# Attention and two feed-forward layers on one core: a second set of probability buffers in the first unit, new instruction orders, short heads' q in two halves

## The reference

```python
scores = scale * np.matmul(q, k.transpose(0, 1, 3, 2)) + bias      # 4 sequences, 8 heads, 576 rows, head_dim 64
scores = scores - np.max(scores, axis=-1, keepdims=True)
attn = np.exp(scores)
attn = attn / (np.sum(attn, axis=-1, keepdims=True) + 1e-09)
x = np.matmul(attn, v)                                             # as 2304 tokens x 512
h = x @ w_in                                                       # layer 1, 512 -> 2048 -> 512
y = (h - np.tanh(h)) @ w_out
g = y @ w_gate                                                     # layer 2, 512 -> 1536 -> 512
out = (g * (1.0 / (1.0 + np.exp(-g))) * (y @ w_val)) @ w_out2
```

## Time and profile before

| | us |
|---|---|
| median of three runs | 1268.38 (1267.01 to 1269.97) |
| the profiled execution's own time | 1264.43 |
| its span, first to last instruction | 1262.6 |
| TensorE busy | 1185.2 (94%) |
| VectorE busy | 635.8 (50%) |
| ScalarE busy | 576.3 (46%) |
| GpSimd busy | 540.2 (43%) |
| mean granted clock of TensorE | 0.991 |

### The profile page before, as it was taken

The page is one execution under the profiler, slowest core; times in us unless marked ns, Lnnn a source line. Parts: engine busy times, 40 slices in busy tenths (PEclk is TensorE's granted clock), DMA queues, the critical chain, the costliest instruction groups (busy, mean ns, idle before and its releaser), DMA issues.

```text
span 1262.6 us, 20294 instructions
## 1 busy us (share of the span) xinstructions
PE 1185.2 (94%) x7312; PEld 1094.9 (87%) x7312; DVE 635.8 (50%) x1401; ACT 576.3 (46%) x1171; POOL 540.2 (43%) x600
## 2 busy tenths in 40 slices
PE   5767699999999999999999999999999999999998
PEld 2346688999999998999899999999999999999998
DVE  8966776666556556777777734521211212112111
ACT  6965566655555555555555544521212222122212
POOL 2046566755555555777777733211111111111111
PEclk9998899999999999999999999999999999999999
DMA  5886455343444433444444334300000001000000
GB/s 176 265 247 181 128 171 178 107 141 104 119 122 129 118 108 117 132 128 128 146 136 127 102 135 147 125 26 1 26 26 25 25 13 39 1 26 1 26 1 26
DMA packets 80068, 125.47 MB, mean 99 GB/s; under 512 B 19424, under 2 KB 42976, under 8 KB 79968
## 3 DMA queue, kind: packets, MB, share of 16 engines
q1 hardware_dynamic: 79968, 124.17, 32.5%
HBM read 104.07 MB, written 20.05 MB: 98 GB/s over the span
## 4 chain that ended last, share of the span: by engine, by line
PE 64%; DVE 18%; issue 8%; ACT 8%; SPq 1%; DMA 1%; DVEq 0%; POOL 0%; ACTq 0%
PE ps_s L1341 12%; PE ps_y L1352 12%; PE ps_y L1271 9%; PE ps_h L1252 8%; PE ps_h L1341 6%; PE ps_pt L1341 6%; DVE prob L993 5%; PE ps_pt L1208 4%; DVE fr L967 3%; DVE feat L960 3%; PE ps_pt L1225 2%; ACT wbuf L738 2%; DVE wbuf L1009 2%; PE ps_s L1192 2%; DVE g_b L1020 2%
## 5 line engine op out<-in xcount | busy, mean ns | idle before, releaser
L669 POOL TENSOR_TENSOR fr<-tanh_b,fr 128x384 fp32r<-128x384 f32 x72 | 73.0, 1014 | 378.1 <-ACT fr L890 378.1
L1271 PE MATMUL ps_y<-fr,wbuf 128*128 128x384 f32 x1152 | 226.2, 337 | 2.0 <-ACT xy_stage L777 1.3
L617 POOL TENSOR_SCALAR prob<-prob,rowinv 128x576 f32<-128x576 f32 (+1 forms) x160 | 127.8, 799 | 207.6 <-DVE rowinv L1004 190.9
L1252 PE MATMUL ps_h<-fr,wbuf 128*128 128x384 f32 x1056 | 206.8, 340 | 1.8 <-DVE g_b L1020 1.8
L1271 PEld LDWEIGHTS ps_y<-fr,wbuf 128*128 128x128 f32 x1152 | 198.8, 188 | 2.6 <-POOL fr L622 2.6
L1252 PEld LDWEIGHTS ps_h<-fr,wbuf 128*128 128x128 f32 x1056 | 182.1, 189 | 3.1 <-DVE g_b L1020 2.8
L731 ACT ACTIVATE prob<-prob,negmax 128x576 f32<-128x576 f32 (+1 forms) x160 | 124.1, 776 | 103.8 <-DVE negmax L993 102.6
L1352 PE MATMUL ps_y<-wbuf,fr 128*128 128x512 f32 x648 | 161.1, 393 | 0.0
L622 POOL TENSOR_TENSOR fr<-g_b,fr 128x384 fp32r<-128x384 f32 x96 | 108.4, 1129 | 110.9 <-ACT fr L755 110.9
L1352 PEld LDWEIGHTS ps_y<-wbuf,fr 128*128 128x128 f32 x648 | 120.5, 188 | 22.1
L1009 DVE TENSOR_TENSOR wbuf<-ps_pt,wbuf 128x512 fp32r<-128x512 f32 (+1 forms) x144 | 97.0, 674 | 58.6 <-ACT wbuf L738 57.5
(11 more groups left out here) (128 smaller groups left out, 1994.9 us busy)
## 6 DMA issues: line engine op xcount, KB each, us to landing
biasb<-bias_scratch SPq DMA_DIRECT2D x128, 216.0 KB, 2.6
raw<-k_t SPq DMA_DIRECT2D x59, 288.0 KB, 2.8
bias_scratch<-w_raw SPq DMA_DIRECT2D x72, 144.0 KB, 3.3
biasb<-bias_scratch SPq DMA_DIRECT2D x64, 144.0 KB, 2.9
w_raw<-w_chunks SPq DMA_DIRECT2D x16, 512.0 KB, 5.4
prob<-w_chunks SPq DMA_DIRECT2D x8, 768.0 KB, 4.2
raw<-v_p SPq DMA_DIRECT2D x32, 160.0 KB, 2.3
biasb<-bias_scratch SPq DMA_DIRECT2D x64, 72.0 KB, 2.6
```

What stands on the lines that cost most here:

```text
L617: eng.tensor_scalar(row, row, rowinv[0:hd.rows, tile % PR:tile % PR + 1], 1.0, ALU.mult, ALU.mult).then_inc(p_norm, 1)
L1252: mm = eng.matmul(hidden_bank(u, c)[:, 0:TOK], w[:, cols], x[:, d, :], start=d == 0 and i == 0, stop=d == KC - 1 and i == 2)
L1271: mm = eng.matmul(ps_y[:, d, 0:TOK], w[:, cols], g[c % 2], start=c == 0 and i == 0, stop=c == C1 - 1 and i == 2)
```

## The change

The probability buffers exist twice in unit 0: even heads below 8 use a second set in a part of `wbuf` that W1 fills later, and `pt_high` waits for the output two heads back. All engines get new orders in the slots of attention alone (`alone`), and the ninth slot (`edge`) finishes head 7 ahead of most of head 8. In the slots of layer 1 with long heads, `q_low` goes ahead of the last `score`, and the W1 splits move: two ahead of the first exponential, two to the slot's end. In a unit's first slot `y_out` is issued in parts. In short slots q of consecutive heads goes to alternating halves of `qq`, so `q_high` and `q_low` come early in the slot, and q is loaded ahead of the bias. In the last unit TensorE runs two hidden chunks ahead of the model chunks rather than one. Near the end of the bias stage, the loads of bias tiles 4 and 5 go ahead of the last two stores of bias.

Buffers and helpers:

```diff
         tail = C1 * 2 * W1C
         k_hi = wbuf[:, tail:tail + S]
...
-        pt_end = wbuf[:, pt_at:pt_at + TOK]
+        pt_bufs = []
+        for pt_at in (tail + S, (C1 - 2) * 2 * W1C):
+            pt_bufs.append([wbuf[:, pt_at + i * FULL * TOK:pt_at + (i + 1) * FULL * TOK] for i in range(2)]
+                           + [wbuf[:, pt_at + 2 * FULL * TOK:pt_at + 2 * FULL * TOK + TOK]])
...
+        def pt_second(hd):
+            return hd.n < H and hd.n % 2 == 0
+        def pt_free(hd):
+            return hd.n - 1 if hd.n < H else hd.n
...
         def operands(hd, moe):
...
+            if not ended(hd):
+                at = hd.n % 2 * width(hd)
+                return qq[:, at:at + width(hd)], k_hi, k_lo
...
+        def preparing_q(hd, moe):
+            if ended(hd) or ended(HEADS[hd.n - 1]):
+                return preparing(hd, moe)
+            return HEADS[hd.n - 1].tile0
```

SyncE's queue:

```diff
             for rnd in range(1, NQUAD, 2):
+                if rnd >= NQUAD - 4:
+                    load_bias(BR + (rnd - (NQUAD - 4)) // 2)
                 store_bias(rnd)
...
-            for n in range(H):
+            load_bias(BR + 2)
+            for n in range(1, H):
...
             for n in range(H, NH):
                 hd = HEADS[n]
                 load_v(hd)
+                following = HEADS[n + 2:n + 3]
+                for nxt in following:
+                    if not ended(hd):
+                        load_q(nxt)
                 for t in range(hd.nt):
+                    if t == 0 and hd.unit > 1 and n == FIRST_OF[hd.unit] + 1:
+                        store_y(hd.unit - 2, 0)
                     load_bias(hd.tile0 + t + BR)
...
+                    if t == 1 and hd.unit > 1 and n == FIRST_OF[hd.unit] + 1:
+                        store_y(hd.unit - 2, 1)
```

GpSimd, the slots of attention alone:

```diff
                 if not moe:
+                    edge = q.n == H
+                    if edge:
+                        split_v(v)
                     if p is not None:
                         split_k(p, moe)
-                    if v is not None:
-                        split_v(v)
                     for t in range(q.nt):
                         norm(q, t)
+                        if t == 0 and v is not None and not edge:
+                            split_v(v)
```

ScalarE:

```diff
+            def alone(q, v, p, moe):
+                for t in range(q.nt):
+                    if v is not None:
+                        pt_high(v, t, moe)
+                    if t == 0 and p is not None:
+                        q_high(p, moe)
+                    exp_tile(q, t)
+                if v is not None:
+                    pt_high_end(v)
+                if q.n >= 2:
+                    o_part(HEADS[q.n - 2], moe)
...
+            def edge(q, v, p, moe):
+                for t in range(v.nt):
+                    pt_high(v, t, moe)
+                o_part(HEADS[v.n - 1], moe)
+                pt_high_end(v)
+                eng.wait_ge(e_score, q.tile0 + 1)
+                x_high(0)
+                exp_tile(q, 0)
+                o_part(v, moe)
+                q_high(p, moe)
+                exp_tile(q, 1)
...
+            def dense_alone(moe):
+                u, s = moe[0][0], moe[0][1] // 2
+                for (u, c), splits in zip(moe, w2_plan(s)):
+                    if c == 0:
+                        y_out(u - 1)
+                    tanh(u, c)
+                    g_high(u, c)
+                    for k in splits:
+                        w2_high(k)
...
+            def short(q, v, p, moe):
...
+                pt_high(v, 0, moe)
+                if first:
+                    y_out(u - 1, [0])
+                if p is not None:
+                    q_high(p, moe)
+                if q is not None:
+                    exp_tile(q, 0)
+                if not first:
+                    tanh(u, c)
+                pt_high(v, 1, moe)
...
+                u, tiles, first = moe[0][0], w1_tiles(moe), begins(moe)
+                pt_high(v, 0, moe)
+                if v.n == H:
+                    exp_tile(v, 2)
+                for k in tiles[-1:] + tiles[0:1]:
+                    w1_high(k)
+                if first:
+                    y_out(u - 1, [0])
+                exp_tile(q, 0)
...
+                o_part(v, moe)
+                if late(moe):
+                    x_high(u + 1)
+                for k in tiles[1:3]:
+                    w1_high(k)
```

VectorE:

```diff
+            def alone(q, v, p, moe):
+                for t in range(q.nt):
+                    score(q, t, moe)
+                    if t == 1 and p is not None:
+                        q_low(p, moe)
+                    if v is not None:
+                        pt_low(v, t, moe)
+                    if t > 0:
+                        inverse(q, t - 1)
+                if v is not None:
+                    pt_low_end(v)
+                if q.n >= 2:
+                    x_out(HEADS[q.n - 2], moe)
+                inverse(q, q.nt - 1)
...
+            def short(q, v, p, moe):
...
+                pt_low(v, 0, moe)
+                if q is not None:
+                    score(q, 0, moe)
+                if p is not None:
+                    q_low(p, moe)
+                if q is not None:
+                    inverse(q, 0)
+                if not first:
+                    gated(u, c)
+                pt_low(v, 1, moe)
+                if q is not None:
+                    score(q, 1, moe)
...
+                x_out(v, moe)
+                if q is not None:
+                    inverse(q, 1)
...
+                pt_low(v, 0, moe)
...
+                score(q, 0, moe)
+                for k in tiles[0:1]:
+                    w1_low(k)
...
+                pt_low(v, 2, moe)
+                if not first:
+                    q_low(p, moe)
+                for t in range(2, q.nt):
+                    score(q, t, moe)
...
+                pt_low_end(v)
...
+                gated(*moe[1])
+                x_out(v, moe)
+                for k in tiles[1:3]:
+                    w1_low(k)
```

TensorE:

```diff
+            def alone(q, v, moe):
+                for t in range(q.nt):
+                    if t == 2 and q.n >= 2:
+                        output(HEADS[q.n - 2], moe)
+                    scores(q, t, moe)
...
+                    if v is not None:
+                        transposed(v, t, moe)
+                if v is not None:
+                    transposed_end(v, moe)
...
+            def edge(q, v, moe):
+                for t in range(v.nt):
+                    transposed(v, t, moe)
+                output(HEADS[v.n - 1], moe)
+                transposed_end(v, moe)
+                scores(q, 0, moe)
+                scores(q, 1, moe)
+                output(v, moe)
+                scores(q, 2, moe)
...
+            def dense_alone(u, c):
+                if c == 0:
+                    pieces = model_pieces(u - 1, C1 - 1) + hidden_pieces(u, 0) + hidden_pieces(u, 1)
+                else:
+                    pieces = (hidden_pieces(u, c) + model_pieces(u, c - 2)
+                              + hidden_pieces(u, c + 1) + model_pieces(u, c - 1))
+                for piece in pieces:
+                    piece()
...
+                gaps = [4, 4, 2] if len(moe) == 2 else [4, 2]
+                if moe[0] == (0, 0):
+                    layer_work(4)
+                    gaps = [0, 0, 2]
```

More of the change, by code:

```diff
@@ new lines, in slot @@
+                g_high(*moe[0])
+                exp_tile(q, 1)
+                if first:
+                    y_out(u - 1, [3])
+                else:
+                    pt_high(v, 2, moe)
+                q_high(p, moe)
+                pt_high_end(v)
+                for t in range(2, q.nt):
+                    exp_tile(q, t)
+                tanh(*moe[1])
+                g_high(*moe[1])
+                o_part(v, moe)
+                if late(moe):
+                    x_high(u + 1)
+                for k in tiles[1:3]:
+                    w1_high(k)
@@ L1108, in slot @@
-                if not one:
-                    x_out(v, moe)
-                for k in tiles[2:3]:
+                    dense_alone(moe)
+                    return
+                if len(moe) == 1:
+                    short(q, v, p, moe)
+                    return
+                u, tiles, first = moe[0][0], w1_tiles(moe), begins(moe)
+                pt_low(v, 0, moe)
+                if v.n == H:
+                    inverse(v, 1)
+                    inverse(v, 2)
+                score(q, 0, moe)
@@ L1123, in _ @@
             eng.sem_inc(v_t, 1)
-            slots(slot, edge)
+            slots(slot)
             def y_low(v, par):
```

357 lines of the change are left out of this document (156 added, 201 removed).

## The result

| | before | after |
|---|---|---|
| median of the runs, us | 1267.70 (1263.24 to 1269.97) | 1247.30 (1247.15 to 1248.48) |
| profiled execution, us (its span) | 1264.43 (1262.6) | 1247.15 (1245.3) |
| mean granted clock | 0.991 | 0.992 |

The ratio is 0.9845, with a 95% interval of 0.9817 to 0.9873: 1.5% faster. The prediction was 1243.4 us, in a range of 1233 to 1256. In the profiled pair the gain is 17.3 us of span, where the sum said 25.0; the medians fell by 20.4.

What follows compares the result with a forecast made beforehand. TensorE was taken as the bound from about 158 us on, with waits left elsewhere, chiefly in attention alone. Gains summed to 25.0 us: 1264.4 - 25.0 = 1239.4 profiled, 1243.4 as a median, range 1233 to 1256.

Steps and rivals of the forecast that it cites:

- Short slots: Short slots of layer 1: early `q_low` stops delaying `x_out`; 28 slots x 0.33 = 9.2 us gained, bounds 0 and 10.
- last unit: Last unit: another hidden chunk covers waits of 1.26 and 0.73 us; 2.3 us gained, bounds 1.5 to 2.6.
- Start: Start of attention alone: earlier load of tile 4's bias saves half of a 4.01 us wait; 2.1 us gained.
- Attention alone: Heads 3 to 7: second buffer set cuts the ring, period 9.09 falls to 8.2 us; 4.5 us gained.
- Ninth slot and edge: Ninth slot and unit 0's first slot: head 7 finished first, some 25 us instead of 28; 2.9 us gained.
- the exposed three: `q_low`, `w1_low` and `x_low`: the only operations listed as open to delay by the port pair VectorE shares with GpSimd.
- Unit 0: Unit 0's six other slots with W1 work: moved W1 splits gain 0.46 of 0.96 us each, 2.8 us.
- the first score chain is as late as before: Unit 0's slots: `w1_low` ahead of the first `inverse` waits for GpSimd's W1 split, limiting the gain to 2.8 us.
- Long slots of units 1 and 2: 14 slots without the two first ones: `q_low` ahead of the third score loses nothing if VectorE gets the ports first; 0.
- rival (a): Long slots: GpSimd gets the ports first every time, output 0.5 us later, 14 slots 7 us, 1250; chance 0.21.
- rival (b): GpSimd keeps the ports over both halves of k, delaying outputs in long slots and unit 0: 40 us, 1283; chance 0.07.
- First slots: First slots of units 1 to 4: `y_out` in parts ends a 0.66 us wait; 1.2 us gained, short units 0.

Runs made afterwards that it cites:

- the run with the stores late: Changed kernel with the last two bias stores (eight issues) moved behind SyncE's loads for head 2; 1248.83 us, ratio 0.986.
- The run with a later `q_low`: Changed kernel with `q_low` in attention alone moved behind the third score's `pt_low` and `inverse`; 1243.86 us, ratio 0.9813.
- the run with `q_low` late: Changed kernel with `q_low` back behind `pt_low_end` in all long slots of layer 1; 1244.47 us, ratio 0.9821.
- the filler: TensorE computes each head's first score four times over in attention alone: on the changed kernel 1246.76 us, on that kernel with three repairs 1250.92 us.

## Why the prediction was right, and where it was not

**Short slots** (9.2, measured 9.0) and **last unit** (2.3, measured 2.6): the mechanism was right in both. The short slots were read off a row of before in which the cost was absent, the last slot without a q; the sum counted 28 of them where there are 27. The two waits of the earlier trace rows in the last unit are gone.

**Start** (2.1, measured 2.6): the size is right, and tile 4 is scored at 77.07, as said. The reason given for the half that stays, the pace of the loads, is half right. At tile 6 VectorE's own chain stands right behind the loads; at tile 7 a bias is still 1.11 us late, which falls into the next term (the run with the stores late). The score of tile 6 came at 83.43 to 85.45 in kernels that start alike, so the 0.5 us over the forecast can't be told from chance.

**Attention alone** (4.5, measured 2.2): the mis-sized term. The period is 8.67, not 8.2. The waiting for the ports was right (0.66 to 0.79 against 0.8); `pt_high_end` is 0.58 instead of 0.3, the clock 0.2 to 0.4 instead of 0.1. With VectorE's 7.0 these make 8.6. The run with a later `q_low` shows that the kernel could have spared 0.72 a slot.

**Ninth slot and edge** (2.9, measured 1.1): the order is worth 2.1 by itself, and 1.0 is lost among the other edits. Part of that is in the first slot of layer 1, where TensorE has four waits of 0.99 to 1.62 us (4.7 in all). The first and the last of them, and what stands before the first on VectorE and GpSimd, in the changed kernel:

```profile
145.57 2.73 PE L1378 MATMUL ps_h<-fr,wbuf 128*128 128x384 f32 x12 [0.99 <-DVE fr L1115]
...
154.43 1.09 PE L1334 MATMUL ps_pt<-ident,prob 128*128 128x128 f32 x4 [1.62 <-DVE wbuf L1086]
...
142.86 2.57 DVE L1115 TENSOR_TENSOR fr<-xy_stage,fr 128x1152 fp32r<-128x1152 f32 x1
...
142.78 1.43 POOL L627 TENSOR_TENSOR fr<-raw,wbuf 128x576 fp32r<-128x576 f32 x1
```

`x_low` begins 0.08 us after GpSimd's low half of k and takes 2.57 us; in the run with the old edge the same instruction takes 1.36. The prediction named `x_low` among the exposed three and put no price on it. TensorE waits 0.99 us for it, so that is the most it can cost. That it does is argued from the rows: no run took it away with the new order kept, and in the run with the later `q_low` the edge takes 30.73 us with an `x_low` just as long, so other waits move it as much. How the gain divides between this term and the one before hangs on the cut: set at head 6's output they are 2.1 and 1.1 us, the other way round. Together they are 3.3 of the 7.4 forecast.

**Unit 0** (2.8, measured 4.8): the step that failed is "the first score chain is as late as before". From a slot's first score to its second `pt_low` the changed kernel takes 2.55 us (192.11 to 194.66) and 2.56 (205.95 to 208.51) in the two kinds of slot, where before it took 3.29 (185.08 to 188.37). The early split does wait for GpSimd in every second slot, but VectorE would have waited for the exponential there, so the first `inverse` is only 0.14 us later. What the prediction said of the splits at the end is half right: in every second slot they and GpSimd's `norm` press on each other, and 0.5 of the 1.0 us is lost again. By the run with `q_low` late, 0.25 of a slot's gain is that of the early `q_low`.

**Long slots of units 1 and 2** (0, measured -3.1): the step that failed is the choice between forecast and rival (a). The prediction's own sign of being wrong, an output in unit 1 that waits for `pt_low_end`, is there in 12 of these 14 slots (0.23 to 0.29 us). GpSimd was first in all 14, by about 0.1 us. The price was 0.35 a slot in ten of them and 0.1 in the last two, where the rival had 0.5; the run with `q_low` late has it back. The second slot of each unit gained 0.35 (14.0 to 13.65). The argument "a waiting VectorE got its turn at once" was right, but it concerns the turn between two instructions of GpSimd, not who is first. It is why rival (b) did not come: GpSimd's low half at 322.83 took 1.60 us behind the waiting `q_low`, where it takes 1.43 with nobody ahead of it.

**First slots** (+1.2, measured -1.3): `y_out` in parts did cut its wait, from 0.66 to 0.20 us, but the change also puts `split_g` behind GpSimd's second `norm` in these slots, and 0.93 us of waiting for it is new. I read that edit and gave it no cost. This step was an omission, not a wrong size. The first two slots of unit 3, taken at 0, lost 0.6: the first output there waits 0.74 us for a `pt_low` where it waited 0.22. No run took that apart.

The Trainium skill (SBUF — State Buffer, SBUF: two separate sides) says that an operation which takes the pair holds it for its whole length. Here the traces agree: `q_low` 0.56 against 1.00 to 1.46, a W1 low half 0.68 against 1.23, and the operations that read PSUM, such as `pt_low` with 0.69 in all of these rows, don't change.

In sum, of 7.7 us by which the span fell short of 25.0, units 1 and 2 hold 5.6 (3.1 and 2.5), attention alone 2.3 and the edge 1.8, and unit 0 gave 2.0 more than forecast. That the median came out 3.9 us from the forecast is in part luck: unit 0's surplus came from a step that the forecast had wrong, and the medians fell by 3 us more than the profiled pair, on which the sum was built.

## What to carry to other kernels

An operation that shares ports with another engine has a price that hangs on who asks first, and here a tenth of a microsecond decided it. When one is moved, list what the other engine runs at its new place, price both orders in each stage apart, and put it where it fills a wait of its own engine; here one `q_low` wanted a different place in attention alone, in unit 0 and in units 1 and 2, and two such moves together with GpSimd's split put first made 10 us more. And give every line of the diff a price, also the reordering of two instructions on an engine that is idle half of the time: its result may be what TensorE waits for.

## What the runs showed of the hardware that I had not expected

The contest for the ports can fall into a pattern: unit 0's slots alternate between 13.37 and 13.85 us through the whole unit, with the same instructions in each, in this kernel and in nine of the runs. It is made at the slot's end, by who is first there, VectorE's two late splits or GpSimd's `norm` (the rows of 189.78 and 203.16). There `norm` takes 0.5 us more where it loses, the splits start 0.1 us later and take 0.2 more where they do. What decides those 0.1 us each time was not settled.

The granted clock of attention alone was 1.00 with the filler in front of TensorE's wait (6.7 us of work in 8.24, a rest of 1.54) and 0.83 with the same filler behind a wait (8.18 in 10.19, a rest of 2.01). That so much work behind a rest doesn't bring the clock back was not expected. The length of the rest does not tell the two apart by itself: in the run with the later `q_low`, slots with rests of 2.29 and 2.44 us had a clock of 1.00, and in the changed kernel the output behind a rest of 3.15 us took 1.64 us and the one behind the next, of 3.13, took 2.20. What decides it was not settled.
